# Two sequences' y turned to tokens by VectorE and through DRAM instead of by TensorE

## The chip, the cores and the metric

One core of one Trainium2 chip. The metric is the time of one execution on the device in microseconds (us); less is better. The core's engines work side by side, each through its own list of instructions in order, and meet only at semaphores: TensorE (PE: matmuls and transposes into PSUM; its weight loads are PEld), VectorE (DVE), ScalarE (ACT), GpSimd (POOL), and SyncE (SP), which here issues every DMA.

## The reference

Windowed attention, a gated layer that mixes tokens, and a mixer with a token layer and a channel layer. All float32, 4 sequences (b) of 576 tokens (s), 512 channels.

```python
# attention: 8 heads of 64, each token sees itself and the 63 before it
attn = softmax(where(mask, q @ k.T / 8, -1e9)) ; x = attn @ v          # (4, 576, 512)
# gated layer
h = relu(x @ w_in); u, v = h[..., :512], h[..., 512:]
v_n = (v - mean(v)) / sqrt(var(v) + 1e-6)
v_s = einsum('ts,bsd->btd', w_spatial, v_n) + b_spatial[None, :, None]
y = (u * v_s) @ w_out                                                   # (4, 576, 512)
# mixer
h = relu(y.transpose(0, 2, 1) @ w_tok1) @ w_tok2                        # over tokens
u2 = y + h.transpose(0, 2, 1)
out = u2 + relu(u2 @ w_ch1) @ w_ch2
```

The step that matters here: y comes out of `w_out` with its channels on the 128 partitions (4 tiles m of 128 channels, 576 tokens along the row), and the first token layer wants tokens on the partitions (5 tiles t, the last of 64 tokens, 512 channels along the row).

## The kernel before

**Arithmetic.** Nearly every product is made of three float32r matmuls on a high and a low part (high x high, high x low, low x high). ScalarE writes the high part of a value, VectorE (or GpSimd) the low part as value minus high part.

**Orders written out.** The work of each engine is a list of names, made of segments: a prologue (attention of sequence 0), a first turn (attention of sequence 1, everything behind it of sequence 0), `LOOP_...` twice (attention of sequence 2 with the rest of sequence 1, then attention of sequence 3 with the rest of sequence 2), and an epilogue. `order_of` turns names into entries; the kinds in `BACK` belong to the sequence before. A digit is a block, a tile, or a tile and a half of the tokens. SP has one list for all, `ALL_SP`, with the sequence as the first digit. In TensorE's list `+` is the second part of the unit before it, so that small pieces can stand between its parts.

**Names, in the order in which the work of a turn depends.** Attention, 9 blocks of 64 queries per sequence: `qt` (DVE turns q by 32x32 blocks; `kt` turns k), `S` (PE, scores), `m` (DVE, mask and maximum), `e` (ACT, exponent), `r` (DVE, inverse of the sum), `n` (POOL, normalise), `pt` (DVE, turn probabilities by 32x32 blocks), `pw` and `pr` (SP, store them to DRAM and load them back with the blocks rearranged: one store, four loads), `V` (PE, values), `o` (ACT, eviction to xT). `V` of a block waits for its `pr`; `pt` of a block waits for the `V` two before it. `lv`, `lk`, `lq` load v, k, q (16 DMAs each for k and q of a later sequence). `vo` copies a window of v. Then `xh`, `xl` (POOL, high and low part of x), `v` and `u` (PE, the two halves of `w_in`), `vr`, `vs`, `rs`, `vn`, `vh`, `vl` (normalising v), `uu` (ACT, u into the tile uy).
Behind it: `g` (PE, mixing over tokens), `sa`, `sm`, `gh`, `gl` (add bias, times u, high, low), `y` (PE, `w_out`), `yy` (ACT, y into uy), `t` (PE, y transposed: four 128x128 transposes of a tile into one PSUM bank), `th`, `tl` (ACT and DVE, high and low part of y by tokens), `a` (PE, first token layer, all tiles into two banks), `ah`, `al`, `b` (PE, second token layer), `te` (DVE, u2 = y + b in uy), `ut` (DVE, u2 turned by 32x32 blocks into `turn_at[m]`), `st` and `sr` (SP, u2 stored as it is, and as rows: the latter with four DMAs for each m that put the blocks in their places). `turn_at[3]` is the tile gate, so the first `sa` of the next turn waits for the last of the row stores.

**PSUM.** Four banks are handed round among the units `v`, `u`, `g`, `y`, `t`, `a`, `b`: a unit takes the bank used longest ago and waits until the unit before it there has been evicted (`take_acc`, `unit_free`).

**Lines.** L1291 is the product of three matmuls, L1392 the same for products over tokens (`over_tokens`: `g` and `a`), L1331 scores, L1361 values, L1310 and L1341 the prologue's transposes, L1380 those of the spatial weights, L1455 the transposes of y. L849 is `th`, L844 `yy`, L1118 `tl`, L1099 `sa`, L1024 `pt`, L1137 `ut`. SP's: L572 `pw`, L578 `pr`, L583 `sr`, L568 `st`, L502 the k and q loads of later sequences, L632 loads of u2 rows in the last stage (channel layer).

Of the kernel before, what the change touches and what calls it, by code (L numbers as in the profile page):

```python
# [25 lines left out]
def bass_attention_gmlp_mixer_kernel(nc, q, k, v, w_in, w_spatial, b_spatial, w_out, w_tok1, w_tok2, w_ch1, w_ch2, out):  # L26
# [21 lines left out]
    def tile_of(blk):  # L48
# [50 lines left out]
        "te30 te01 vn0 vs1 te11 vl0 te21 te31 vn1 ut0 vs2 ut1 vl1 vn2 vs3 vl2 vn3 ut2 ut3 vs4 kt0 vl3 vn4 kt1 vl4").split()  # L99
# [10 lines left out]
        "n0 n1 n2 n3 n4 xh0 n5 n6 xh1 xl0 n7 xl1 n8 xh2 xl2 rs0 rs1 xh3 xl3 xh4 xl4 rs2 rs3 rs4").split()  # L110
# [9 lines left out]
        "cw40 cw41 st30 st31 st32 st33 ca42 sr30 sr31 sr32 sr33").split()  # L120
# [23 lines left out]
    BACK = ("g", "y", "t", "a", "b", "sa", "sm", "gh", "gl", "yy", "th", "tl", "ah", "al", "te", "ut")  # L144
# [40 lines left out]
    with ctx:  # L185
# [144 lines left out]

        prob_dram = nc.dram_tensor("prob_blocks", (2, 4, P, P), F32, kind="Internal").ap()
# [19 lines left out]
        a_low = sem("a_low")  # L351
        w2_low = sem("w2_low")
# [77 lines left out]
        ODD = counts(DVE_ORDER, ("vo",))  # L430

# [321 lines left out]
        def _(act):  # L753
# [196 lines left out]
        def _(dve):  # L950
# [654 lines left out]
```

## Time and profile before

| | |
|---|---|
| time, median of 3 runs | 655.45 us (653.43 to 655.53) |
| the profiled execution | 653.59 us, of which the span of its instructions 651.0 us |
| granted clock of TensorE | 1.00 in the whole span |
| PE busy | 638.4 us, 98% of the span |
| DVE, ACT, POOL busy | 433.1, 297.8, 138.4 us |
| DMA | 76.76 MB over the one queue that SP fills, 45.2% of 16 engines' time |

The span runs from the first to the last instruction. Busy time leaves out waits and the issuing of DMAs. A chain that ended last is followed back from the last instruction, at each step to what released it. Rows of a timeline begin with the start and the length in us; `x4` is a count of instructions, and what stands in square brackets is idle time of the engine just before the row and what ended it.

### The profile page before, as it was taken

The page shows a single profiled execution, that of the slowest core. Times are in us where ns is not written, and L with a number is a line of the kernel's source. Part 1 is how long each engine was busy: PE and PEld are TensorE (multiplying, and loading weights), DVE is VectorE, ACT ScalarE, POOL GpSimd, SP SyncE. Part 2 cuts the span into 40 slices and gives each one's busy share as a digit, 9 for nine tenths or more (in the row PEclk, how much of TensorE's full clock was granted, in tenths as well). Part 3 has the DMA queues.
Part 4 walks back from the last instruction along what each step waited for, and adds up shares of the span by engine and source line. Part 5 has one row for each costly group of instructions (what it writes and reads, how often), then busy time and mean ns, then how long its engine had stood idle before and what let it go on. Part 6 is the DMA issues. An engine that isn't in the chain of part 4 may idle for free.

```text
span 651.0 us, 11538 instructions
## 1 busy us (share of the span) xinstructions
PE 638.4 (98%) x3917; PEld 589.1 (90%) x3917; DVE 433.1 (67%) x1073; ACT 297.8 (46%) x733; POOL 138.4 (21%) x232
## 2 busy tenths in 40 slices
PE   5899999999999999999999999999999999999997
PEld 5798999989998899988999989988898889889886
DVE  4988887666865778766473666776756775755534
ACT  4865447334464344652347334453334454243331
POOL 3561426531234304252107700000000000000000
PEclk9999999999999999999999999999999999999999
DMA  9858135586444883344730174252632332422412
GB/s 209 212 92 197 35 86 158 129 169 107 128 117 116 178 139 87 107 121 113 165 128 2 61 177 134 73 173 83 213 108 65 121 107 64 163 64 66 162 33 97
DMA packets 190872, 77.48 MB, mean 119 GB/s; under 512 B 127328, under 2 KB 177056, under 8 KB 190816
## 3 DMA queue, kind: packets, MB, share of 16 engines
q1 hardware_dynamic: 190816, 76.76, 45.2%
q8 instruction: 32, 0.52, 0.3%
q14 instruction: 24, 0.20, 0.1%
HBM read 55.49 MB, written 21.23 MB: 118 GB/s over the span
## 4 chain that ended last, share of the span: by engine, by line
PE 95%; DMA 2%; DVE 1%; POOL 1%; SPq 0%; issue 0%; ACT 0%; POOLq 0%; DVEq 0%
PE ps L1291 71%; PE ps L1392 13%; PE ps L1361 4%; PE ps L1331 4%; DMA early<-in_moe_w_spatial_dram 2%; PE ps L1455 1%; PE ps L1310 0%; PE ps L1380 0%; DMA out_dram<-front 0%; DVE front L1195 0%; PE ps L1341 0%; DVE att L995 0%; ACT att L763 0%; POOL att L675 0%; SPq L544 0%
## 5 line engine op out<-in xcount | busy, mean ns | idle before, releaser
L1291 PE MATMUL ps<-arena 128*128 128x288 f32 (+3 forms) x2100 | 396.3, 342 | 0.0
L1291 PEld LDWEIGHTS ps<-arena 128*128 128x128 f32 (+1 forms) x2100 | 335.2, 186 | 33.7
L1291 PE MATMUL ps<-att_r,arena 128*128 128x384 f32 x504 | 101.5, 336 | 0.0
L1291 PEld LDWEIGHTS ps<-att_r,arena 128*128 128x128 f32 x504 | 90.0, 188 | 7.1
L1392 PE MATMUL ps<-arena 128*128 128x288 f32 (+1 forms) x560 | 89.6, 316 | 0.0
L1392 PEld LDWEIGHTS ps<-arena 128*128 128x128 f32 x560 | 80.5, 188 | 4.1
L690 POOL TENSOR_SCALAR att<-att,rinv 128x128 f32<-128x128 f32 x144 | 53.8, 393 | 98.1 <-DVE rinv L1006 97.9
L783 ACT ACTIVATE att<-att,nmax 128x128 f32<-128x128 f32 x144 | 56.0, 392 | 25.8 <-DVE nmax L995 25.3
L881 ACT ACTIVATE xT<-ps 128x384 f32<-128x384 f32 x54 | 26.5, 491 | 52.1 <-PE ps L1291 52.1
L1171 DVE TENSOR_TENSOR arena<-front,arena 128x1792 fp32r<-128x1792 f32 x16 | 32.4, 2025 | 16.1 <-ACT arena L873 16.0
L1181 DVE TENSOR_TENSOR vr<-ps,xT 128x384 f32<-128x384 f32 x36 | 20.0, 556 | 31.7 <-PE ps L1291 25.0
L995 DVE CUSTOM_DVE_ANT_0 att<-ps,mask 128x128 f32<-128x128 f32 x144 | 33.1, 285 | 11.5 <-PE ps L1331 11.0
L893 ACT ACTIVATE arena<-vr 128x384 fp32r<-128x384 f32 x36 | 18.7, 520 | 43.8 <-PE ps L1291 35.7
L1331 PE MATMUL ps<-att 128*128 128x128 f32 x288 | 37.4, 280 | 0.9 <-DVE att L969 0.9
L1361 PE MATMUL ps<-att 128*128 128x128 f32 x288 | 37.1, 276 | 0.7 <-DVE att L969 0.4
L873 ACT ACTIVATE arena<-front 128x1792 fp32r<-128x1792 f32 x18 | 30.7, 1704 | 13.4 <-DVE front L1161 13.4
L1186 DVE SCALAR_TENSOR_TENSOR arena<-vr,arena 128x384 fp32r<-128x384 f32 x36 | 21.2, 589 | 23.3 <-ACT arena L893 23.3
L1331 PEld LDWEIGHTS ps<-att 128*128 128x128 f32 x288 | 35.4, 196 | 1.3 <-DVE att L969 1.2
L1361 PEld LDWEIGHTS ps<-att 128*128 128x128 f32 x288 | 34.7, 192 | 1.7 <-DVE att L969 0.6
L793 ACT ACTIVATE xT<-ps 64x256 f32<-64x256 f32 x72 | 27.1, 377 | 14.6 <-PE ps L1361 13.6
L893 ACT ACTIVATE arena<-xT 128x384 fp32r<-128x384 f32 x18 | 9.5, 525 | 48.4 <-PE ps L1291 32.7
L1129 DVE TENSOR_TENSOR uy<-ps,uy 128x288 f32<-128x288 f32 x32 | 14.2, 454 | 20.4 <-PE ps L1291 20.3
(101 smaller groups left out, 651.8 us busy)
## 6 DMA issues: line engine op xcount, KB each, us to landing
front<-in_moe_w_ch_dram SPq DMA_DIRECT2D x18, 512.0 KB, 4.7
prob_blocks<-att SPq DMA_DIRECT2D x27, 256.0 KB, 2.5
att<-prob_blocks SPq DMA_DIRECT2D x108, 64.0 KB, 2.0
u_scratch<-uy SPq DMA_DIRECT2D x16, 288.0 KB, 2.9
front<-in_moe_w_ch_dram SPq DMA_DIRECT2D x18, 256.0 KB, 2.9
front<-in_moe_w_ch_dram SPq DMA_DIRECT2D x36, 128.0 KB, 3.5
early<-u_rows SPq DMA_DIRECT2D x18, 256.0 KB, 5.6
att<-in_v_dram SPq DMA_DIRECT2D x16, 256.0 KB, 3.8
```

Source lines behind the costliest of these rows:

```text
L690: ins = pool.tensor_scalar(x, x, rinv[:, g % 3, p:p + 1], 1.0, ALU.mult, ALU.mult)
L783: ins = act.activation(x, x, ACT.Exp, bias=nmax[:, g % 3, p:p + 1], scale=-1.0, accum_out=psums[:, g % 3, p:p + 1])
L793: ins = act.activation(xT3[c, :, blk * WINDOW:(blk + 1) * WINDOW], tp[c, bank, :].rearrange("p (w h n) -> p w h n", w=PAIRS, h=2)[:, :, h, ...
L873: act.activation(a_hi_at[n % 2], a_raw[n % 2], ACT.Copy).then_inc(a_hi, 1)
L881: act.activation(part[x], ps[:, 6, 0:CK], ACT.Copy).then_inc(part_copied, 1)
L893: act.activation(h_at[:, j, 0], total[i], ACT.Relu).then_inc(h_hi, 1)
L995: ins = dve.tensor_tensor_reduce(out=prob[:, g % 3, P * p:P * (p + 1)], in0=ps[:, 4 + g % 2, P * p:P * (p + 1)], in1=mask[:, 0:P] if blk e ...
L1171: dve.tensor_tensor(a_lo_at[n % 2], a_raw[n % 2], a_hi_at[n % 2].bitcast(F32), ALU.subtract).then_inc(a_low, 1)
L1291: ins = pe.matmul(dst, w[a], x[c], start=first and n == 0, stop=last and n == 2, skip_group_check=True)
L1331: ins = pe.matmul(ps[:, 4 + g % 2, P * p:P * (p + 1)], qd[:, g // 2 % 2, g % 2, p].rearrange("p h n -> p (h n)"), kT[:, p, at:at + P], sta ...
L1361: ins = pe.matmul(tp[:, bank, P * p:P * (p + 1)], window[:, P * p:P * (p + 1)], keys[:, p], start=True, stop=True)
L1392: ins = pe.matmul(dst, d, w, start=t == 0 and n == 0, stop=t == NT - 1 and n == len(pairs) - 1, skip_group_check=True)
```

## The change

Sequences 1 and 2 (second and third, `TURNED`) no longer have `t` in TensorE's list. In its place: `ty` (DVE turns the 576 columns of uy's tile m by 32x32 blocks into `turn_at[m]`), `yw` (SP, four DMAs for each m that store the blocks to rows of `y_dram`, 72 KB each in pieces of 128 B), `yr` (SP, one DMA for each tile t that loads rows of 2 KB into `raw_y`, once all of y is stored and the last `g` is done). `raw_y` lies where the low part of vn lies, so `tl` works in place. `th` and `tl` read it instead of PSUM. The first sequence and the fourth keep TensorE's transposes. The orders of both loop turns are written anew for all engines, and `ALL_SP` from its start. The prologue, first turn and epilogue of the other engines are unchanged.

```diff
     LOOP_PE = (
-        "g00 S0 S1 + g10 S2 S3 + g20 + g30 + g01 + g11 + g21 + g31 S4 S5 V0 V1 + y00 + y10 + y20 + y30 + y01 S6 "
-        "V2 t0 + y11 + y21 + y31 + t1 S7 V3 t2 S8 V4 t3 t4 a0 a1 a2 a3 v0 a4 V5 V6 + v1 + b00 b10 b20 b30 b01 b11 "
-        "V7 V8 b21 v2 + b31 v3 + v4 + u00 + u10 + u20 + u30 + u01 + u11 + u21 + u31 +").split()
+        "S0 S1 g00 + g10 S2 + g20 + g30 + g01 + g11 + S3 S4 V0 g21 + g31 + y00 + y10 + V1 S5 V2 y20 + y30 + y01 + "
+        "y11 + S6 V3 y21 + y31 + V4 S7 v0 + S8 v1 V5 + a0 a1 a2 a3 a4 V6 v2 + b00 b10 b20 b30 b01 V7 b11 b21 V8 "
+        "b31 v3 + v4 + u00 + u10 + u20 + u30 + u01 + u11 + u21 + u31 +").split()
...
     LOOP_ACT = (
...
+        "e0 e1 e2 gh00 gh10 gh20 gh30 e3 gh01 e4 o0 gh11 gh21 yy00 yy10 gh31 o1 yy20 yy30 yy01 e5 yy11 o2 yy21 o3 "
+        "yy31 e6 e7 vr0 o4 th0 th1 o5 th2 th3 th4 vr1 e8 ah0 ah1 vh0 o6 vr2 o7 o8 vh1 vh2 vr3 uu00 vr4 uu10 vh3 "
+        "uu20 uu30 uu01 vh4 uu11 uu21 uu31").split()
...
     LOOP_DVE = (
...
+        "qt0 qt1 qt2 m0 qt3 m1 qt4 r0 m2 sa00 r1 pt0 sa10 sm00 sm10 pt1 gl00 gl10 sa20 sa30 sm20 r2 qt5 m3 sm30 "
+        "gl20 pt2 sa01 gl30 sm01 r3 m4 sa11 vo1 gl01 r4 sa21 sm11 pt3 sm21 gl11 pt4 sa31 sm31 gl21 gl31 qt6 m5 "
+        "ty0 vo2 r5 ty1 m6 pt5 ty2 qt7 ty3 qt8 r6 m7 pt6 r7 m8 vs0 tl0 tl1 pt7 tl2 tl3 tl4 vo3 vn0 r8 al0 al1 pt8 "
+        "vl0 vs1 te00 vn1 te10 te20 te30 te01 vo4 te11 kt0 te21 te31 ut0 ut1 vs2 vn2 ut2 vl1 vl2 vs3 ut3 vs4 kt1 "
+        "vn3 vn4 vl3 vl4").split()
...
     LOOP_POOL = (
-        "n0 n1 n2 n3 n4 xh0 n5 n6 xh1 xl0 n7 xl1 n8 xh2 xl2 rs0 rs1 xh3 xl3 xh4 xl4 rs2 rs3 rs4").split()
+        "n0 n1 n2 n3 n4 n5 xh0 xl0 xh1 n6 xl1 n7 xh2 rs0 xl2 n8 rs1 xh3 xl3 xh4 xl4 rs2 rs3 rs4").split()
...
     ALL_SP = (
-        "lq00 lk00 lq01 lv00 lv01 lk01 lq02 lk02 lw01 lq03 lk03 lv02 lw00 lw02 lz04 lv03 lk10 lv04 lq10 lw06 lv10 "
...
+        "lq00 lk00 lq01 lv00 lk01 lv01 lq02 lk02 lw01 lq03 lv02 lk03 lw00 lw02 lv03 lz04 lv04 lk10 lq10 lw04 lw06 "
...
+        "pw17 pw18 pr17 pr18 lk20 st00 st01 st02 st03 lq20 sr00 sr01 sr02 sr03 pw20 lv20 pr20 pw21 lv21 pw22 pr21 "
+        "pr22 lv22 pw23 pw24 pr23 pr24 yw10 lv23 yw11 pw25 yw12 yw13 pr25 pw26 yr10 yr11 yr12 yr13 yr14 pr26 pw27 "
+        "lk30 pw28 pr27 lv24 pr28 st10 lq30 st11 sr10 st12 st13 sr11 sr12 lv30 sr13 pw30 pr30 pw31 lv31 pw32 pr31 "
+        "pr32 pw33 pw34 lv32 pr33 pr34 yw20 yw21 pw35 yw22 yw23 pr35 yr20 yr21 yr22 yr23 yr24 pw36 lv33 pr36 pw37 "
+        "lv34 pr37 pw38 pr38 st20 st21 st22 cx40 cx41 cx42 sr20 st23 cx43 sr21 sr22 sr23 ca40 ca41 cw40 st30 st31 "
+        "sr30 sr31 sr32 sr33 ca42 st32 st33 cw41").split()
...
+                if kind == "yw":
+                    sp.wait_ge(y_turned, Y_TURNED["ty", b, x])
+                    for i in range(4):
+                        sp.dma_start(y_dram[b % 2, :, x * P + 32 * i:x * P + 32 * i + 32].rearrange("(j p) n -> p j n", p=32),
+                                     turn_at[x][32 * i:32 * i + 32, :].rearrange("p (j n) -> p j n", n=32)).then_inc(y_stored[x], 16)
+                if kind == "yr":
+                    if x == 0:
+                        for m in range(KD):
+                            sp.wait_ge(y_stored[m], 64 * b)
+                        sp.wait_ge(*unit_full(("g", b, 31)))
+                    sp.dma_start(raw_y[0:rows(x), 1, x], y_dram[b % 2, toks(x), :]).then_inc(y_in[x], 16)
...
             def yt_high(b, t):
                 r = rows(t)
-                act.wait_ge(*unit_full(("t", b, t)))
-                act.activation(vn[0:r, 0, t, :], ps[0:r, BANK_OF["t", b, t], :], ACT.Copy).then_inc(yt_hi, 1)
+                if b in TURNED:
+                    act.wait_ge(y_in[t], 16 * b)
+                    src = raw_y[0:r, 1, t]
+                else:
+                    act.wait_ge(*unit_full(("t", b, t)))
+                    src = ps[0:r, BANK_OF["t", b, t], :]
+                act.activation(vn[0:r, 0, t, :], src, ACT.Copy).then_inc(yt_hi, 1)
...
+            def turn_y(b, m):
+                dve.wait_ge(rows_stored[m], 64 * b)
+                apart(dve)
+                dve.wait_ge(*unit_free(("y", b, 10 * m + 1)))
+                dve.transpose(turn_at[m], uy3[:, m, :]).then_inc(y_turned, 1)
```

## Rows read from the trace of the kernel before

**Rows 1.** The page: busy times, GB/s of 40 slices, chain by engine

```profile
PE 638.4 (98%) x3917; PEld 589.1 (90%) x3917; DVE 433.1 (67%) x1073; ACT 297.8 (46%) x733; POOL 138.4 (21%) x232
...
GB/s 209 212 92 197 35 86 158 129 169 107 128 117 116 178 139 87 107 121 113 165 128 2 61 177 134 73 173 83 213 108 65 121 107 64 163 64 66 162 33 97
...
PE 95%; DMA 2%; DVE 1%; POOL 1%; SPq 0%; issue 0%; ACT 0%; POOLq 0%; DVEq 0%
```

**Rows 2.** The chain in order of time, third sequence's turn (start, length)

```profile
152.61 1.18 PE ps L1392 x9
...
159.21 11.15 PE ps L1392 x84
...
172.14 1.79 PE ps L1361 x16
...
183.50 0.44 PE ps L1455 x4
183.94 5.60 PE ps L1291 x42
...
194.86 5.49 PE ps L1392 x24
...
204.41 8.88 PE ps L1291 x54
...
237.66 1.18 PE ps L1392 x9
```

**Rows 3.** TensorE's timeline of the start

```profile
12.45 0.66 PE L1310 MATMUL ps<-ident,att 128*128 128x128 f32 x4 [0.99 <-DMA att<-in_k_dram]
...
30.05 1.09 PE L1380 MATMUL ps<-ident,early 128*128 128x128 f32 x8 [0.33 <-DMA early<-in_moe_w_spatial_dram]
```

**Rows 4.** VectorE's groups by form, 150 to 240 us (busy us, mean ns)

```profile
L1118 DVE TENSOR_TENSOR arena<-ps,arena 128x512 fp32r<-128x512 f32 x4 | 2.7, 684 | 2.0 <-ACT arena L849 2.0
...
L1137 DVE STREAM_TRANSPOSE early<-uy 128x576 f32<-128x576 f32 x3 | 2.3, 775 | 0.0
```

**Rows 5.** VectorE's timeline, start of the same turn

```profile
161.98 0.46 DVE L1099 TENSOR_TENSOR gate<-ps,bias 128x288 f32<-128x288 f32 x1 [0.99 <-DMA u_rows<-gate]
162.36 0.70 DVE L1024 STREAM_TRANSPOSE att<-att 128x512 f32<-128x512 f32 x1
```

**Rows 6.** SP's timeline, 125 to 182 us (length is that of the issues)

```profile
126.99 9.36 SPq L502 DMA_DIRECT2D att<-in_k_dram  x16
...
138.50 10.63 SPq L502 DMA_DIRECT2D att<-in_q_dram  x16
149.18 6.62 SPq L583 DMA_DIRECT2D u_rows<-early  x12
...
163.08 0.38 SPq L572 DMA_DIRECT2D prob_blocks<-att  x1
...
165.61 3.88 SPq L578 DMA_DIRECT2D att<-prob_blocks  x8
```

**Rows 7.** DMA issues, 150 to 240 us (KB each, median us to landing)

```profile
prob_blocks<-att SPq DMA_DIRECT2D x9, 256.0 KB, 2.5
att<-prob_blocks SPq DMA_DIRECT2D x36, 64.0 KB, 2.0
u_rows<-early SPq DMA_DIRECT2D x23, 72.0 KB, 2.1
att<-in_v_dram SPq DMA_DIRECT2D x5, 256.0 KB, 3.4
```

**Rows 8.** The page's DMA issues, of the last stage

```profile
front<-in_moe_w_ch_dram SPq DMA_DIRECT2D x18, 256.0 KB, 2.9
...
early<-u_rows SPq DMA_DIRECT2D x18, 256.0 KB, 5.6
```

**Rows 9.** ScalarE's groups by form, 150 to 240 us

```profile
L844 ACT ACTIVATE uy<-ps 128x288 f32<-128x288 f32 x8 | 3.3, 408 | 3.4 <-PE ps L1291 3.4
...
L849 ACT ACTIVATE arena<-ps 128x512 fp32r<-128x512 f32 x4 | 2.4, 597 | 2.6 <-PE ps L1455 2.6
```

More of the change, by code:

```diff
@@ L78, in bass_attention_gmlp_mixer_kernel @@
     LOOP_ACT = (
-        "e0 e1 e2 gh00 gh10 gh20 e3 gh30 gh01 e4 gh11 yy00 o0 o1 yy10 yy20 gh21 gh31 yy30 o2 yy01 th0 e5 yy11 e6 "
-        "yy21 yy31 th1 th2 o3 th3 e7 o4 e8 th4 ah0 o5 ah1 vr0 o6 vr1 vh0 o7 o8 vr2 vh1 vr3 vh2 uu00 vr4 vh3 uu10 "
-        "uu20 uu30 uu01 uu11 vh4 uu21 uu31").split()
+        "e0 e1 e2 gh00 gh10 gh20 gh30 e3 gh01 e4 o0 gh11 gh21 yy00 yy10 gh31 o1 yy20 yy30 yy01 e5 yy11 o2 yy21 o3 "
+        "yy31 e6 e7 vr0 o4 th0 th1 o5 th2 th3 th4 vr1 e8 ah0 ah1 vh0 o6 vr2 o7 o8 vh1 vh2 vr3 uu00 vr4 uu10 vh3 "
+        "uu20 uu30 uu01 vh4 uu11 uu21 uu31").split()
     EPILOGUE_ACT = (
@@ L95, in bass_attention_gmlp_mixer_kernel @@
     LOOP_DVE = (
[3 rows of a table removed]
-        "te30 te01 vn0 vs1 te11 vl0 te21 te31 vn1 ut0 vs2 ut1 vl1 vn2 vs3 vl2 vn3 ut2 ut3 vs4 kt0 vl3 vn4 kt1 vl4").split()
[4 rows of a table added]
+        "vn3 vn4 vl3 vl4").split()
     EPILOGUE_DVE = (
@@ L113, in bass_attention_gmlp_mixer_kernel @@
     ALL_SP = (
[6 rows of a table removed]
-        "cw40 cw41 st30 st31 st32 st33 ca42 sr30 sr31 sr32 sr33").split()
[7 rows of a table added]
+        "sr30 sr31 sr32 sr33 ca42 st32 st33 cw41").split()
     SEGMENTS = {"PE": [PROLOGUE_PE, FIRST_PE, LOOP_PE, LOOP_PE, EPILOGUE_PE], "ACT": [PROLOGUE_ACT, FIRST_ACT, LOOP_ACT, LOOP_ACT, EPILOGUE_ACT],
@@ L143, in bass_attention_gmlp_mixer_kernel @@
     AHEAD = ("kt",)
-    BACK = ("g", "y", "t", "a", "b", "sa", "sm", "gh", "gl", "yy", "th", "tl", "ah", "al", "te", "ut")
+    BACK = ("g", "y", "t", "a", "b", "sa", "sm", "gh", "gl", "yy", "th", "tl", "ah", "al", "te", "ut", "ty")
     PE_ORDER, ACT_ORDER, DVE_ORDER, POOL_ORDER = (order_of(e) for e in ("PE", "ACT", "DVE", "POOL"))
@@ L329, in bass_attention_gmlp_mixer_kernel @@
         rows_dram = nc.dram_tensor("u2_rows", (B * S, DM), F32, kind="Internal").ap()
+        y_dram = nc.dram_tensor("y_rows", (2, S, DM), F32, kind="Internal").ap()
         prob_dram = nc.dram_tensor("prob_blocks", (2, 4, P, P), F32, kind="Internal").ap()
@@ L351, in bass_attention_gmlp_mixer_kernel @@
         a_low = sem("a_low")
+        y_turned = sem("y_turned")
+        y_stored = [sem(f"y_stored{i}") for i in range(KD)]
+        y_in = [sem(f"y_in{i}") for i in range(NT)]
         w2_low = sem("w2_low")
@@ L430, in bass_attention_gmlp_mixer_kernel @@
         ODD = counts(DVE_ORDER, ("vo",))
+        Y_TURNED = counts(DVE_ORDER, ("ty",))
+        TURNED = (1, 2)
+        raw_y = early[:, START["vn"] - START["w_out"]:START["tok2"] - START["w_out"]].rearrange("p (s t n) -> p s t n", s=2, t=NT)
         def unit_full(u):
@@ L856, in token_high @@
                     for m in range(3):
-                        act.wait_ge(rows_stored[m], 64 * b)
+                        if b in TURNED:
+                            act.wait_ge(y_stored[m], 64 * b)
+                        else:
+                            act.wait_ge(rows_stored[m], 64 * b)
                 act.wait_ge(*unit_full(("acc_a", b, c)))
@@ L1117, in yt_low @@
                 dve.wait_ge(yt_hi, YT_HI["th", b, t])
-                dve.tensor_tensor(vn_low(t), ps[0:r, BANK_OF["t", b, t], :], vn[0:r, 0, t, :].bitcast(F32), ALU.subtract) \
+                src = raw_y[0:r, 1, t] if b in TURNED else ps[0:r, BANK_OF["t", b, t], :]
+                dve.tensor_tensor(vn_low(t), src, vn[0:r, 0, t, :].bitcast(F32), ALU.subtract) \
                     .then_inc(acc_dve, 1)
@@ L1135, in turn_residual @@
                     dve.wait_ge(rows_stored[m], 64 * b)
+                if b in TURNED:
+                    dve.wait_ge(y_stored[m], 64 * b)
                 dve.wait_ge(acc_dve, ACC_DVE["te", b, 10 * m + 1])
@@ L1217, in _ @@
                     spatial_lo(x)
+                elif kind == "ty":
+                    turn_y(b, x)
                 elif kind == "vs":
```

9 rows, old and new, of tables (ALL_SP, LOOP_DVE) are left out of this document.

## The prediction, made before the change was run

> **What bounds the kernel now.** I read the page first, for the busy shares and the chain that ended last. TensorE is busy 638.4 of 651.0 us and the chain is 95% its own work [rows 1]: any instruction taken off TensorE is worth its full time, and any wait put before it costs its full time, unless something else is already late. Second, the chain of waits in order of time, over the turn of the loop in which attention of the third sequence is woven with the gated and token layers of the second [rows 2]: from 152.61 to 237.66 us there is no piece that isn't TensorE's. I count times in a turn from its start (+0 is 152.61). The same rows price TensorE's pieces: a tile's four y transposes 0.44, one block of scores or values 0.89 (x16 is two blocks), a `g` unit of 14 matmuls 1.86 (11.15 x 14 / 84), a `y` or `u` unit of 12 matmuls 1.60, less in longer rows (I take 1.58), a `b` unit half of that, a `v` unit 2.73 and a step of `a` 1.37, its last somewhat less. Third, TensorE's timeline of the start, where its few waits are [rows 3]. Then I walk the other engines in their new written order, with the durations of the rows below.
>
> **What goes.** Ten tiles of y (five in each of two turns) lose their four transposes: 10 x 0.44 = 4.4 us less on TensorE [rows 2]. ScalarE's and VectorE's evictions stay in number, with another source. By itself this is -4.4 us.
>
> **What comes, and where it lies.** For each of two sequences: 4 block transposes on VectorE of 0.78 us [rows 4] = 3.1 us; 16 stores of 72 KB and 5 loads of up to 256 KB on SP's queue. An issue of the same stores took 6.62 / 12 = 0.55 us [rows 6], of the loads about 0.44 (a 256 KB store's 0.38 and a 64 KB load's 0.485 are the nearest rows [rows 6]). That is 16 x 0.55 + 5 x 0.44 = 11 us more in SP's order per turn. VectorE has room in sum, SP too; what counts is each due time on TensorE.
>
> **Place 1: the first values block, turn one.** `V0` stood at +19.5 [rows 2]; in the new order it stands after 6 `g` units and 5 blocks of scores: 6 x 1.86 + 5 x 0.89 = +15.6. What feeds it doesn't move. `pt0` stands behind `sa00` on VectorE, and `sa00` is held by the previous sequence's last row store until 161.98 us (+9.4), by a wait of 0.99 us [rows 5]. The work before that point is untouched, so `pt0` again ends near +10.85 (now r1's two small instructions are ahead of it too); `pw20` is issued at +10.9; its read-back may go 2.53 us later (165.61 - 163.08 [rows 6]), at +13.4; the fourth of its loads is issued 3 x 0.485 later and lands 2.0 us after that [rows 6, 7]: +16.9. A wait of 1.3 us, where before 2.5 us were to spare. Bounds 1.0 (shortest landings) to 1.5. Queued behind `V0` is all of TensorE. `g01`, due at +10.1, needs `sa00`, done at +9.85: it just passes. In turn two the row stores were issued much earlier, so neither binds.
>
> **Place 2: y to tokens.** Between the end of `y31` and `a0` TensorE has `V4 S7 v0 S8 v1 V5`: 4 x 0.89 + 2 x 2.73 = 9.0 us. In turn one `y31` ends at +38.7 (with place 1's wait) and `a0` is due at +47.8. The chain: eviction by ScalarE 0.41 [rows 9], `ty3` 0.78 behind `qt7`, done at +40.05. SP is later than that: it waits for the third sequence's `ty1` and `ty2`, and `pw25` lies between, so `yw12` is issued from +38.5, `yw13` from +40.6 to +42.7. Then `pr25` (four issues, 1.75) and `pw26` (0.4) stand ahead of `yr10`: +44.85. The last store landed (2.1 after its issue [rows 7]) at +44.3, so the queue, not the landing, sets it. The load is 256 KB: the nearest rows are 2.9 us for a load of that size with long rows and 3.4 with short ones [rows 7, 8]; I take 2.9, then `th0` 0.60 [rows 9] and `tl0` 0.68 [rows 4]: `a0` can start at +49.2, a wait of **1.4 us**. `V5`, due 1.4 us before it, also waits for `pr25` about 0.6 us, which is inside the same 1.4. Later tiles come 0.44 to 0.7 us apart, `a` steps take 1.37, so no further wait. In turn two there is no `pw36` ahead of the loads: `yr20` goes at +43.05, `a0` could start at +47.35 against +46.35 due: **1.0 us**. Bounds for each: a landing of 2.0 (the shortest kind, 64 KB) takes 0.9 off; one of 5.6, as the same rows-to-tokens loads took in the last stage, where six queued behind each other and behind weights [rows 8], adds 2.7. I stand by 2.9 because here the queue is drained before them.
>
> [...]
>
> **Place 3: `V7` and `V8`, turn one.** The k load of the next sequence, 16 DMAs that took SP 9.36 us [rows 6], moves ahead of `pw28` and `pr27`. `pt7` waits for `tl1`, so `pw27` goes at +50.6 and the k load from +51.0 to about +60.2; `pw28` +60.6, `pr27` to +62.3, landed +63.9. `V7` is due at +63.3: 0.6. `pr28` follows by 2.5 and the `V` before it by one more wait of about 0.1. I take 0.7; bounds 0 and 1.8 (landings of 3 us behind that burst). In turn two the k load isn't there: 0.
>
> **Place 4: the start.** SP's first loads change order too. `lv01` now lies between the k and q tiles that TensorE waits for (0.99 us, for the third k tile), which may cost up to 1.2 (its 256 KB at the 212 GB/s of that slice [rows 1]); `lv02` moves ahead of `lk03`, so the spatial weights are asked for 0.6 us sooner, which can give back the 0.33 wait [rows 3]. Together 0, bounds -0.3 and +1.2.
>
> **Hidden.** The q load now lies ahead of the u2 stores `st11` to `st13` in turn one (16 issues, 10.6 us [rows 6]): `uu10` comes about 2 us late, but its bank is needed only 2.5 us after that; by my walk `u31` has 1.5 us to spare. `sa31`, due for the bank of `y30`, has 0.25 us. If that cover is gone, each costs what it is late. GpSimd's new order lets `xh0` wait for `y31` before `n6`; `n6` is still done before `pt6` is wanted. The order written for TensorE from 322.70 us on is the same.
>
> **The sum.** -4.4 + 1.3 + 1.4 + 1.0 + 0.7 + 0 = 0.0 us (with each wait at its least, 0.3 + 1.8 + 0.7 + 0.3 lower, -3.1; at its most, 0.2 + 5.4 + 1.1 + 1.2 higher, +7.9). Against the profiled execution's own 653.59 us (a span of 651.0 and 2.6 around it) that is 653.6. The median shown is 655.45, two runs near 655.5 and one at 653.43, so the profiled one was among the quick ones; I put the sum on the median: 655.4 us. 0.3%, or 2.0 us, is about what a measurement can tell from no change.
>
> **The rivals.**
> *A, the trip is hidden and the gain is kept (faster).* If the y stores go at 0.40 apiece (a single issue took 0.38 [rows 6]) instead of 0.55, the eight of `yw12` and `yw13` save 1.2 us and `yr10` goes at +43.6; with a landing of 2.5, as the 256 KB store's, `a0` is on time in both turns. If the row store behind `sa00` also lands 0.6 us sooner, place 1 is halved. -4.4 + 0.7 + 0 + 0 + 0.3 is -3.4: 652.0. For it: TensorE shows no wait in the old turns, so waits of this kind were avoided throughout. Against it: the +9.4 release and the 2.53 us between store and read-back are rows, not guesses. It decides from a sum of waits under 2.4 us.
> *B, the loads of y queue (slower).* All five loads are issued at once, 1.2 MB, and the first shares the engines with them, with `pr25` and with the last stores. If the first lands after 5.6 us as in [rows 8], each `a0` waits 2.7 us more: 0.0 + 5.4 = 660.8; with 4.2 us, 658.0. It decides from a landing of 3.9 us. For it: that very kind of load has no shorter row. Against it: those stood behind 1.5 MB of weights.
> The Trainium skill (VectorE: DVE Perf Modes, Rules for kernel authors) advises TensorE for a 128x128 transpose and VectorE only for 32x32 ones; it points to B's side, and no row here decides it.
> *C, nothing is taken off the path.* It would need TensorE to idle where the transposes stood; it doesn't [rows 1, 2], so only the waits above can eat the gain.
>
> **Chances.** No measurable change, the sum as it stands, 0.50. A, faster, 0.28. Slower 0.22: B with 0.15, late covers (`u31`, `y30`, place 3 at its bound) 0.07. The range takes in A whole and B up to a landing of about 4.4 us: 651.0 to 658.5, which leaves out less than 2 in 10. My own likeliest case spans 653.5 to 657.4.
>
> **What would show it.** Right: L1455 falls from 80 to 40 matmuls; VectorE has 8 more transposes of 128x576; in TensorE's waits, one of about 1.3 us on the att load before `V0` only in turn one, two of 1 to 1.5 us on VectorE's low part before `a0`, one under 1 us before `V7`; both turns of about equal length as before, the first some 1 us longer, the second 1 us shorter. Wrong: a y load that lands in over 4 us or under 2.5, no wait at `V0`, or a wait in the run of `u` units.

## The result: 2.4% slower

| | before | after |
|---|---|---|
| time, median of 6 runs each | 653.08 us (651.71 to 655.53) | 669.51 us (668.01 to 670.2) |
| ratio, 95% interval | | 1.0241 [1.0216, 1.0266] |
| the profiled execution | 653.59 us, span 651.0 | 669.25 us, span 667.4 |
| TensorE busy | 638.4 us | 639.2 us |
| mean granted clock | 1.00 | 0.994 |

The change costs 16.4 us; the forecast was 655.4 us with a range to 658.5. The page of the changed kernel answers to [rows 1]: busy times of the engines, GB/s of 40 slices, the chain by engine.

```profile
PE 639.2 (96%) x3877; PEld 586.3 (88%) x3877; DVE 444.0 (67%) x1081; ACT 298.7 (45%) x733; POOL 138.4 (21%) x232
...
GB/s 212 208 106 170 32 100 166 114 180 115 147 143 195 156 117 111 149 183 199 139 35 1 59 222 84 63 159 73 211 126 88 85 143 64 156 66 64 157 32 95
...
PE 78%; SPq 9%; DMA 7%; DVE 2%; issue 2%; ACT 2%; POOL 1%; DVEq 0%; POOLq 0%; ACTq 0%
```

Forty matmuls are gone and eight block transposes are there, as the change says, yet TensorE is busy for no less time: a part ran at half clock (below), and a piece right behind a wait counts longer (1.16 for 1.05). The chain was 95% TensorE's and is now 78%; SP's issuing (SPq), which had 0%, has 9%. So the place to look is SP's queue. TensorE's timeline says where the time went. I cut it at TensorE's first unit of each turn (the first `g` in the old order, the first scores in the new one) and at the start of the epilogue.

| stretch | before | after | difference | predicted |
|---|---|---|---|---|
| start to turn one | 152.45 | 152.47 | 0.0 | 0 |
| turn one | 85.05 | 90.04 | +5.0 | +1.2 |
| turn two | 85.05 | 85.59 | +0.5 | -1.2 |
| epilogue to the end of the span | 328.5 | 339.3 | +10.8 | 0 |

**Turn one.** TensorE's timeline of the changed kernel, the middle of the turn (L1402 values, L1372 scores, L1332 three-part products, L1433 products over tokens, here `a`; a wait of the row stands in square brackets):

```profile
190.75 1.06 PE L1372 MATMUL ps<-att 128*128 128x128 f32 x8
192.26 3.02 PE L1332 MATMUL ps<-arena 128*128 128x512 f32 x12 [0.45 <-POOL arena L730]
...
200.31 1.16 PE L1402 MATMUL ps<-att 128*128 128x128 f32 x8 [2.76 <-DMA att<-prob_blocks]
...
203.70 4.66 PE L1433 MATMUL ps<-arena 128*128 128x512 f32 x18 [0.84 <-DVE arena L1149]
208.90 2.58 PE L1433 MATMUL ps<-arena 128*128 128x512 f32 x10 [0.54 <-DVE arena L1149]
...
222.49 1.16 PE L1402 MATMUL ps<-att 128*128 128x128 f32 x8 [0.71 <-DMA att<-prob_blocks]
```

The largest wait is not `a0`'s for y (0.84) but that of `V5` for its probabilities, 2.76 us, shortly before it. SP's timeline of the same kernel shows why (start and length of the issues; L594 is `yw`, the y stores, L589 `pr`, L583 `pw`, L601 `yr`, L550 `lv`):

```profile
184.73 3.38 SPq L594 DMA_DIRECT2D y_rows<-early  x4
188.21 0.46 SPq L550 DMA_DIRECT2D att<-in_v_dram  x1
188.71 2.47 SPq L594 DMA_DIRECT2D y_rows<-early  x4
191.22 0.51 SPq L583 DMA_DIRECT2D prob_blocks<-att  x1
191.78 2.65 SPq L594 DMA_DIRECT2D y_rows<-early  x4
194.47 2.21 SPq L594 DMA_DIRECT2D y_rows<-gate  x4
196.73 1.96 SPq L589 DMA_DIRECT2D att<-prob_blocks  x4
198.73 0.43 SPq L583 DMA_DIRECT2D prob_blocks<-att  x1
199.34 2.36 SPq L601 DMA_DIRECT2D early<-y_rows  x5
```

From 184.7 us on SP does nothing but issue. `pw25` went at 191.22, and its read-back could have gone some 2.5 us later (as `pr20` did behind `pw20`), but the eight stores `yw12` and `yw13` stand between them and hold it until 196.73. The sixteen stores took 10.7 us, not 8.8: 0.84 each for the first four as a mean, then 0.62, 0.66, 0.55. Then the loads of y: ScalarE's timeline (L876, `th`), with what it waited for.

```profile
202.29 0.63 ACT L876 ACTIVATE arena<-early 128x512 fp32r<-128x512 f32 x1 [5.66 <-DMA early<-y_rows]
203.75 0.63 ACT L876 ACTIVATE arena<-early 128x512 fp32r<-128x512 f32 x1 [0.83 <-DMA early<-y_rows]
```

The first load landed 2.9 us after its issue, as I took it; the other four, all five issued within 2.36 us, landed 4.0, 4.6, 5.7 and 5.6 us after their issues, so up to 1.6 us apart, and that is the 0.54 before a later step of `a`.

**Turn two** has only 0.45 at `v0` and 1.15 at `V5`; no `pw36` lies ahead of its y loads.

**Last stage.** The chain of waits in order of time, start and length, where the last stage (L1332 again) stops:

```profile
371.92 6.29 PE ps L1332 x43
...
379.08 0.78 DVE early L1176
...
379.88 0.32 SPq L605
...
388.32 0.53 SPq L605
...
388.95 0.48 SPq L617
...
390.03 3.43 DMA front<-in_moe_w_ch_dram
...
395.07 1.70 ACT arena L903
396.77 0.39 ACT xT L911
...
397.30 6.78 PE ps L1332 x26
```

Read from its end: TensorE waits 7.58 us (390 to 397) for ScalarE (L911), which stands behind the high part of channel weights (L903), which waits for VectorE's sums of them, and these for three loads, issued from 388.95 on (the last at 390.03) behind sixteen row stores `sr30` to `sr33` (L605), the first of which waited for u2 of the last sequence turned by VectorE, done at 379.86. Before, the same weights (`ca42`, L595 to L597) had gone ahead of the row stores. SP's timeline of the kernel before:

```profile
373.64 0.41 SPq L595 DMA_DIRECT2D front<-in_moe_w_ch_dram  x1
374.10 0.57 SPq L596 DMA_DIRECT2D front<-in_moe_w_ch_dram  x1
374.72 0.46 SPq L597 DMA_DIRECT2D front<-in_moe_w_ch_dram  x1
375.22 7.29 SPq L583 DMA_DIRECT2D u_rows<-early  x12
```

That is one edit at the very end of `ALL_SP`: its first row store stands 88 us behind the last `a0` that reads a y from DRAM (291.37). The windows of the changed kernel there (busy us and instructions of PE, PEld, DVE, ACT, POOL; then clock, DMA share, GB/s):

```profile
388.00:392.00 4.00, 1.72 (x8) 1.10 (x7) 0.00 (x0) 0.00 (x0) 0.00 (x0) 1.00 0.72 166
392.00:396.00 4.00, 0.00 (x0) 0.00 (x0) 1.52 (x4) 0.93 (x1) 0.00 (x0) 0.70 0.91 295
396.00:400.00 4.00, 2.71 (x8) 2.64 (x9) 2.60 (x3) 2.77 (x5) 0.00 (x0) 0.50 0.89 281
400.00:404.00 4.00, 4.00 (x20) 3.59 (x20) 2.74 (x5) 0.76 (x2) 0.00 (x0) 0.94 0.37 131
```

After 7.6 us of idleness TensorE resumes at a granted clock of 0.50, 1.2 GHz, and is back near full speed in the next window. From the start of the epilogue to the end of TensorE's last matmul lie 335.8 us against 325.0: 10.8, of which 7.58 is this wait, 1.26 another at 588.56 (below), and most of the rest, 2.0, the slow clock: the first two groups behind the wait (397.30 to 401.25) took 3.95 us in place of 2.43.

### The profile page after: what moved, and what is told of

It reads as the page before. It is cut to its first block, busy times and chain, and to the rows that moved or that the text cites. A ratio compares the mean times of both kernels' runs of the same rounds, so it can differ in the third digit from the quotient of the medians.

```text
span 667.4 us, 11510 instructions
## 1 busy us (share of the span) xinstructions
PE 639.2 (96%) x3877; PEld 586.3 (88%) x3877; DVE 444.0 (67%) x1081; ACT 298.7 (45%) x733; POOL 138.4 (21%) x232
## 4 chain that ended last, share of the span: by engine, by line
PE 78%; SPq 9%; DMA 7%; DVE 2%; issue 2%; ACT 2%; POOL 1%; DVEq 0%; POOLq 0%; ACTq 0%
PE ps L1332 59%; PE ps L1433 11%; PE ps L1402 3%; SPq L594 3%; PE ps L1372 3%; SPq L589 2%; DMA prob_blocks<-att 2%; DMA front<-in_moe_w_ch_dram 1%; DMA early<-in_moe_w_in_dram 1%; SPq L605 1%; SPq L513 1%; DMA early<-y_rows 1%; DMA att<-prob_blocks 1%; DVE front L1234 1%; PE ps L1382 1%
## 5 line engine op out<-in xcount | busy, mean ns | idle before, releaser
L1332 PE MATMUL ps<-arena 128*128 128x288 f32 (+3 forms) x2100 | 399.3, 343 | 0.9 <-POOL arena L730 0.9
L1332 PEld LDWEIGHTS ps<-arena 128*128 128x128 f32 (+1 forms) x2100 | 335.5, 187 | 34.9 <-POOL arena L730 1.3
L1332 PE MATMUL ps<-att_r,arena 128*128 128x384 f32 x504 | 102.7, 339 | 8.8 <-ACT xT L911 8.8
L1332 PEld LDWEIGHTS ps<-att_r,arena 128*128 128x128 f32 x504 | 90.7, 189 | 16.5 <-issue 9.7
L1433 PE MATMUL ps<-arena 128*128 128x288 f32 (+1 forms) x560 | 89.6, 316 | 1.5 <-DVE arena L1149 1.4
L1433 PEld LDWEIGHTS ps<-arena 128*128 128x128 f32 x560 | 80.2, 188 | 7.2 <-DVE arena L1149 3.3
L805 ACT ACTIVATE att<-att,nmax 128x128 f32<-128x128 f32 x144 | 56.2, 392 | 23.5 <-DVE nmax L1025 23.1
L911 ACT ACTIVATE xT<-ps 128x384 f32<-128x384 f32 x54 | 26.6, 492 | 52.6 <-PE ps L1332 52.6
L1402 PE MATMUL ps<-att 128*128 128x128 f32 x288 | 38.4, 277 | 5.4 <-DMA att<-prob_blocks 5.1
L1402 PEld LDWEIGHTS ps<-att 128*128 128x128 f32 x288 | 35.3, 191 | 7.7 <-DMA att<-prob_blocks 6.6
L903 ACT ACTIVATE arena<-front 128x1792 fp32r<-128x1792 f32 x18 | 30.7, 1704 | 22.8 <-DVE front L1200 22.8
L1372 PE MATMUL ps<-att 128*128 128x128 f32 x288 | 38.4, 283 | 0.6 <-DVE att L999 0.6
L1372 PEld LDWEIGHTS ps<-att 128*128 128x128 f32 x288 | 36.4, 199 | 1.1 <-DVE att L999 0.8
L861 ACT ACTIVATE arena<-gate 128x288 fp32r<-128x288 f32 x32 | 13.8, 445 | 31.7 <-DVE gate L1136 31.6
```

Source lines behind the costliest of these rows:

```text
L805: ins = act.activation(x, x, ACT.Exp, bias=nmax[:, g % 3, p:p + 1], scale=-1.0, accum_out=psums[:, g % 3, p:p + 1])
L903: act.activation(a_hi_at[n % 2], a_raw[n % 2], ACT.Copy).then_inc(a_hi, 1)
L911: act.activation(part[x], ps[:, 6, 0:CK], ACT.Copy).then_inc(part_copied, 1)
L1332: ins = pe.matmul(dst, w[a], x[c], start=first and n == 0, stop=last and n == 2, skip_group_check=True)
L1372: ins = pe.matmul(ps[:, 4 + g % 2, P * p:P * (p + 1)], qd[:, g // 2 % 2, g % 2, p].rearrange("p h n -> p (h n)"), kT[:, p, at:at + P], sta ...
L1402: ins = pe.matmul(tp[:, bank, P * p:P * (p + 1)], window[:, P * p:P * (p + 1)], keys[:, p], start=True, stop=True)
```

## The experiments

Theories at the start. T1: SP's order is the cause, in two places: its end (the 9 to 10 us of the last stage) and the y stores ahead of `pr25` and the y loads (turns one and two). T2, the rival: the cost lies in the trip itself, its landings and the memory traffic, and in the turns' other new orders, so restoring one piece of SP's list gives little. All times are medians; ratios are to the kernel before on the same chip, with a 95% interval.

**1. The changed kernel with the old end of SP's list.**

```diff
-... ca40 ca41 cw40 st30 st31 sr30 sr31 sr32 sr33 ca42 st32 st33 cw41
+... ca40 ca41 cw40 cw41 st30 st31 st32 st33 ca42 sr30 sr31 sr32 sr33
```

> The changed kernel with only the end of SP's list put back: st30 to st33 and then ca42 (the third set of channel weights) ahead of the sixteen row stores sr30 to sr33. Theory (late weights): the last stage lost 10.9 us because ca42 stood behind the row stores; of it 7.6 us are the wait at 389.7 us, about 2 the half clock after it, 1.3 a second weight load at 587 us. Expected 658.6 to 660 us, 9.6 to 10.9 less than the changed kernel, about 1.008 to 1.010 of the kernel before. Rival (the trip through DRAM itself delays the last stage, by DMA traffic or by the last turn): no more than 3 us come back, 666 to 670.

Measured: 659.69 us (657.62 to 660.66), 1.0096 [1.0065, 1.0127]. Epilogue and last stage take 325.0 us again, the clock is 0.999. So the end of the list was 9.8 of the 16.4 us, as expected, and 6.4 are left: turn one 89.4 us, turn two 86.9. (Turn two had 85.6 in the changed kernel's profile, with the same orders: a turn moves by over 1 us from one profile to the next.) The edit also moves `cw41`, `st32` and `st33`; it is `ca42` that the chain above names.

**2. The kernel before with only the new end of SP's list** (the same words the other way round, y still transposed by TensorE).

> The kernel before with only the end of SP's list as in the changed kernel: ca42 behind sr33, st32 st33 cw41 last; nothing of y is changed. Theory (late weights): it alone costs 9.6 to 10.9 us, 663 to 664.5, with one wait of 7 to 8 us before the second group of hidden units and a half clock of TensorE after it. Rival (it needs the new turns): no change, 653.

Measured: 662.19 us (661.86 to 662.58), 1.0136 [1.0118, 1.0153]: +8.9, somewhat less than expected. TensorE's timeline of this kernel:

```profile
381.19 1.22 PE L1291 MATMUL ps<-att_r,arena 128*128 128x384 f32 x6
382.25 1.55 PE L1291 MATMUL ps<-arena 128*128 128x512 f32 x6
391.22 2.26 PE L1291 MATMUL ps<-att_r,arena 128*128 128x384 f32 x6 [7.42 <-ACT xT L881]
393.28 2.03 PE L1291 MATMUL ps<-arena 128*128 128x512 f32 x6
395.15 1.22 PE L1291 MATMUL ps<-att_r,arena 128*128 128x384 f32 x6
```

The same wait without anything of y's trip, and the price of the clock in plain sight: six matmuls that took 1.22 us take 2.26 right after the wait, and the next six 2.03 instead of 1.55; the rows after are normal. Its epilogue and last stage are 9.2 us longer: 7.42 and 1.7 more, 1.5 of it in the two groups right behind the wait. T1 holds for this place, from both sides.

**3 and 4. One turn of each kind** (both with the old end): the y trip and the new orders in one turn, the kernel before's orders and TensorE's transposes in the other.

```diff
-        TURNED = (1, 2)
+        TURNED = (2,)         # run 3: only turn two is new
...
+        TURNED = (1,)         # run 4: only turn one is new
```

> End of SP's list as before; the first of the two loop turns with the old orders and TensorE's transposes, the second with the new orders and the trip through DRAM (third sequence only). Theory (two costs, one for each turn, that don't depend on each other): +0.5 us against before, as the trace of the changed kernel has 85.6 us for that turn against 85.05, so 653.5 to 654. Rival (a turn in the new order pays for what the first new turn left late): the second turn alone would gain up to 2.2, 651.

> The mirror of e3: only the first loop turn new (second sequence's y through DRAM), the second turn and the end of SP's list old. Theory: +5.0 us against before (90.04 against 85.05 us for that turn), 658 to 658.5. Rival (the wait before a0 is a chance of the profiled run): between 0 and +2.5.

Measured: turn two alone 656.16 us (655.61 to 658.32), 1.005 [1.0031, 1.007]; turn one alone 659.31 us (657.7 to 662.28), 1.0097 [1.0063, 1.013]. In the profiles turn one is 4.5 us longer where it alone is new (89.5), turn two 1.15 longer where it alone is (86.2), and the old turn beside it keeps its 85.0. Both came out above what I expected, and turn two's trip isn't free. The profile of run 3 has a wait of 2.24 us at 402.46 in the last stage as well, on weights that landed late (8.5 us for 128 KB), and epilogue and last stage are 4.0 us longer there; that of run 4 has one of 0.98 at 404.46.

Run 4's TensorE timeline shows a second price of a wait in the turn:

```profile
199.16 2.08 PE L1418 MATMUL ps<-att 128*128 128x128 f32 x8 [2.25 <-DMA att<-prob_blocks]
200.88 2.33 PE L1348 MATMUL ps<-arena 128*128 128x512 f32 x6
```

The same two pieces took 1.16 and 1.64 behind `V5`'s wait in the changed kernel. The granted clock of this stretch is 0.70 (200 to 204 us), against 1.00 there, though the changed kernel waited longer, 2.76. So waits of this size sometimes bring the half level and sometimes don't: in run 4 three of four executions had a mean clock of 0.995 to 0.997, in run 3 one of five, in run 1 two of four; before is at 0.999 to 1.00 throughout. The losses of the halves sum to 8.8 us in place of 6.4. Such episodes can't explain all of it: in run 3 four of five executions, the median among them, had a clock of 1.00. The intervals of the three runs, about 1.3, 2.2 and 2.0 us to either side, barely leave room for no difference; the rest stays open.

**5. The orders alone.** Everything of run 1, but no `ty`, `yw`, `yr`; TensorE's transposes are put into its new list.

```diff
-y11 + S6 V3 y21 + y31 + V4 S7 v0 + S8 v1 V5 + a0 a1 a2 a3 a4 V6 ...
+y11 + S6 V3 y21 + y31 + V4 t0 S7 t1 v0 t2 + S8 v1 V5 + t3 t4 a0 a1 a2 a3 a4 V6 ...
```

> The new orders of both turns, end of SP's list as before, but y of the second and third sequence transposed by TensorE as before (t0, t1, t2 among V4, S7, v0; t3, t4 ahead of a0), with no trip through DRAM. Theory (the new orders by themselves cost next to nothing, the trip costs it): 653.5 to 655, with v0 and V7, V8 waiting 0.5 to 1.5 us in all. Rival (the new orders are worse whatever carries y): 657 or more.

Measured: 654.25 us (653.58 to 657.3), 1.0014 [1.0003, 1.0025]. Both turns take 85.66 us with no wait that the timeline names; 0.6 more than the old ones. (The profile is that of the slowest execution, 657.3 us; its epilogue and last stage are 3.0 us longer than before's.) By the interval the new orders cost 0.2 to 1.6 us.

**6. The orders, the block transposes and the stores of y, read by nobody.** Run 5 and `ty` and `yw`; `yr` is left out, and `th` and `tl` read TensorE's transposes. It prices VectorE's and SP's load without the dependence of `a` on it (`ah0` and `ut` still wait until the stores have landed, as in the changed kernel).

```diff
+ty0 vo2 r5 ty1 m6 pt5 ty2 qt7 ty3 tl0 ...             # VectorE
+... yw10 lv23 yw11 pw25 yw12 yw13 pr25 pw26 pr26 ...  # SP
```

> As e6, and VectorE also turns y by blocks and SP also stores it to DRAM (16 stores for each of the two sequences), which nothing reads; the tokens come from TensorE's transposes. It separates the load on SP's queue from the wait for the trip. Theory (SP's queue holds up the probabilities' loads behind the stores): a wait before V5 of 1 to 1.5 us in the first turn and up to 0.5 in the second, 1 to 2 us over e6. Rival (only the dependence of a0 on the trip costs): the same as e6.

Measured: 656.98 us (656.16 to 659.25), 1.0055 [1.0038, 1.0073]: 2.7 us above run 5, more than either side expected. In its profile (again the slowest execution) turn one takes 88.2 us and turn two 86.1. TensorE's timeline of it, where the large wait was:

```profile
199.16 1.16 PE L1402 MATMUL ps<-att 128*128 128x128 f32 x8 [1.03 <-DMA att<-prob_blocks]
...
219.79 1.16 PE L1402 MATMUL ps<-att 128*128 128x128 f32 x8 [0.69 <-DMA att<-prob_blocks]
```

and `V5` in TensorE's timeline of run 5:

```profile
197.99 1.05 PE L1401 MATMUL ps<-att 128*128 128x128 f32 x8
```

`V5` waits for `pr25` although nothing of the attention depends on y: the stores delay it by sitting ahead of it in SP's queue. `pr25` was issued at 195.57 us, in run 5 at 190.27, and landed 1.9 to 2.2 us after its issues, no later than elsewhere. The stores also load the DMA engines, which are 82% busy from 184 to 196 us for 150 GB/s; without the stores (run 5) 29% for 79 GB/s.

**7. A second queue for the last y stores.** Half of `yw2` and `yw3` issued by ScalarE, and the y loads ahead of `pw26`.

```diff
-for i in range(4):                     # SP
+for i in range(4 if x < 2 else 2):
...
+yy31 yw2 yw3 e6 e7 vr0 ...             # ScalarE issues i = 2, 3
...
-yw12 yw13 pr25 pw26 yr10 yr11 yr12 yr13 yr14 pr26
+yw12 yw13 pr25 yr10 yr11 yr12 yr13 yr14 pw26 pr26
```

> As e1 (end of SP's list restored), and of the stores of y those of the last two channel tiles shared out: two of four on SP's queue, two on ScalarE's, with the y loads now ahead of pw26. Theory (the trip is late because SP issues sixteen stores one after another at about 0.6 us): the y loads go 3 us sooner in the first turn, the values block V5 no longer waits (2.5 us in e1), a0 waits about 1 us; turns of 86.2 and 84.1 us, 653.5 in all. Rival (the landing of the five loads behind each other sets a0 and a3, whenever they are issued): V5's wait goes, but as much comes back at a0 and a3, 656 to 657.

Measured: 664.38 us (661.84 to 666.05), 1.0164 [1.0143, 1.0186]: 4.7 us worse than run 1 where a gain was expected. `V5` and `a0` no longer wait, as I wanted. But two other waits of turn one, 2.21 us at `v1` (for `xl1`) and 2.98 at `V7`, were each followed by a stretch at half clock, here the second one in TensorE's timeline:

```profile
220.18 2.08 PE L1410 MATMUL ps<-att 128*128 128x128 f32 x8 [2.98 <-DMA att<-prob_blocks]
221.91 3.23 PE L1340 MATMUL ps<-arena 128*128 128x288 f32 x12
```

The twelve matmuls took 1.84 us at full clock in the changed kernel. The mean clock was 0.991 to 0.995 in all five executions. Both waits are explained with the next run, which has them too.

**8. Every y store split between both queues.** As run 7, with half of each `yw`, and ScalarE's earlier in its order.

> As e5 with all four tiles' stores shared between SP's and ScalarE's queue, eight issues each. Theory: y loads go near 195 us in the first turn, a0 is on time; what is left of waits are v0 on GpSimd's low part (0.45 in each turn) and V7, V8 (0.85 in the first). 650.5 to 651.5, 0.996 to 0.997 of the kernel before: this is the version that could beat it. Rival (the trip's landings): 654 or more. A second rival: ScalarE is held by the issues, yy and e6 come late, and a wait of 1 us or more shows before V6 or S8.

Measured: 660.3 us (659.34 to 662.26), 1.011 [1.0092, 1.0128]. What I wanted happened: SP issues the y loads at 196.42, 2.9 us sooner than in the changed kernel, and neither `a0` nor `V5` waits in turn one. ScalarE's timeline tells what it cost (ACTq is ScalarE's DMA issues; L805 is `e`):

```profile
189.94 1.21 ACTq L871 DMA_DIRECT2D y_rows<-early  x2
191.19 2.08 ACTq L871 DMA_DIRECT2D y_rows<-gate  x2
193.32 0.40 ACT L805 ACTIVATE att<-att,nmax 128x128 f32<-128x128 f32 x1 [2.97 <-issue]
```

and TensorE's where it arrives:

```profile
192.13 3.06 PE L1340 MATMUL ps<-arena 128*128 128x512 f32 x12 [0.45 <-POOL arena L730]
...
198.30 1.65 PE L1340 MATMUL ps<-arena 128*128 128x512 f32 x6 [2.22 <-POOL arena L730]
...
220.75 1.16 PE L1410 MATMUL ps<-att 128*128 128x128 f32 x8 [4.20 <-DMA att<-prob_blocks]
```

`e6` stands 2.97 us behind ScalarE's issues; `n6` is late by it, and behind `n6` in GpSimd's order stands `xl1`, for which `v1` waits 2.22 us. The wait of `V7` comes from `pw26`, which now stands behind the y loads: issued at 198.76, it landed 5.3 us later (in run 7 5.2; ahead of the loads 2.7 in the changed kernel and 2.8 in run 1). SP waited for it until 204.13 before it could issue `pr26`, so `pw27` and the sixteen k loads (206.39 to 215.06) went no sooner than in the changed kernel, though TensorE was 2.5 us ahead; `pr27` was issued at 216.76 in place of 215.44, and `V7` waits 4.20 us, with a granted clock of 0.50 from 222 to 224. The second rival's mechanism, ScalarE held by its issues, came true, with the wait at `v1`; the late `pw26` was in no expectation.

**9. The k and q loads moved out of the way.** The k load of the next sequence behind `pr28`, the q load issued by ScalarE late in the turn.

```diff
-pw27 lk30 pw28 pr27 lv24 pr28 st10 lq30 st11 ...
+pw27 pr27 pw28 lv24 pr28 lk30 st10 st11 ...           # the q load by ScalarE
```

> As e1 with only the k and q loads of the next sequence changed as in e9; y stores all on SP. Theory (the k load ahead of pw28 costs what e1's profile shows at V7 and V8): 0.85 us less than e1, 658.5 to 659, all in the first turn. Rival: q on ScalarE's queue delays uu and costs 1 us or more.

Measured: 660.23 us (658.13 to 661.79), 1.0104 [1.0084, 1.0125]: no gain over run 1 where 0.85 us was expected. `V7` no longer waits, but `V0` waits 0.48, `V8` 0.87 and a `u` unit 0.60.

**10. Run 9, and some of the y stores to ScalarE (`yw0` whole, `yw1` half), `xl1` ahead of `n6`.**

> A version made from what e1, e5 and e7 showed: end of SP's list as before; of the y stores, tile 0 and half of tile 1 on ScalarE's queue while it is idle, the rest on SP; GpSimd's xl1 ahead of n6; the next sequence's k load behind pr28, its q load (16 DMAs) on ScalarE's queue in pairs among its later work. Theory (each wait was SP's queue, or an engine held by issues): v1 no longer waits on GpSimd (2.2 us in e7), V7 no longer behind the k load (4.2 in e7), a0 waits under 1 us, v0 0.45 in each turn. 650 to 651.5, 0.995 to 0.997. Rival (the trip's own latency, two landings in a row and the loads that share the engines, leaves 1.5 to 2 us at a0 and a3 in each turn): 653 to 655, no gain over the kernel before.

Measured: 662.99 us (660.15 to 664.65), 1.0141 [1.0113, 1.017]. It was to be the version that beats both kernels, and even its rival (653 to 655) was too low. In turn one most of the waits that I went for became smaller (`V5` 1.55 against 2.51 in run 1; none at `v0`, `v1` or `V7`), `a0`'s did not (1.02 against 0.80), and others came. TensorE's timeline:

```profile
191.12 1.16 PE L1391 MATMUL ps<-att 128*128 128x128 f32 x8 [0.74 <-DVE att L1027]
...
202.42 6.64 PE L1452 MATMUL ps<-arena 128*128 128x512 f32 x28 [1.02 <-DVE arena L1168]
...
233.61 9.76 PE L1351 MATMUL ps<-arena 128*128 128x288 f32 x60 [2.18 <-ACT vr L843]
```

The granted clock is 0.62 from 234 to 238 us, behind the last. The 2.18 us comes from the moved k load: sixteen issues from 215.66 on now last 11.67 us, the stores of u2 stand behind them, and ScalarE waits 4.52 us for one of those before it may overwrite uy. No version that I ran beats the kernel before.

Of the two theories, T1 holds at the end of SP's list (runs 1 and 2) and for `pr25` behind the y stores (run 6). T2 has a part as well: run 5 prices the new orders at 0.7 us, and runs 7 and 8 show a landing that the trip's own loads delay.

## Why the prediction was wrong

**The step that failed: "Hidden", its last sentence.** It says that the order written for TensorE from 322.70 us on is the same, and the sum takes that as a last stage of the same length. TensorE's order is the same; SP's isn't, and the diff shows it: `ca42` behind `sr30` to `sr33`. Most of it could have been read from before's trace: those row stores took 7.3 and 2.2 us of issues from 375.22 on, so a load behind them goes 9.5 us later; the high part of these weights was done at 381.30 and the group of matmuls that needs it began at 384.01, so 2.7 us were to spare, and a wait of 6.8 us is an estimate from these rows (7.58 measured). I walked SP's list in turn one and not its end. This was 9.8 us of 16.4 (run 1 against the changed kernel), 8.9 by itself (run 2). It was none of the rivals; "an edit far from the place that the change is about" was in no chance.

**"What goes", 4.4 us:** right in number (L1455, now L1496, from 80 matmuls to 40). The bill of the rest, without the end, follows from runs 5, 6 and 1, each against the kernel before on its chip (+0.7, +3.4, +6.4): orders 0.7, VectorE's and SP's load 2.7, then the dependence on the trip in place of the transposes 3.0. The last holds the 4.4 us that the transposes give back, so depending on the trip costs about 7.4 by itself, and the trip with its load 10.1 for 4.4 gained. The turns in the profiles of these runs give 1.2, 3.0 and 2.0 for the three; the step from run 6 to run 1 is the least sure, as their intervals (1.0038 to 1.0073 and 1.0065 to 1.0127) touch.

**Place 1:** predicted 1.3, measured 0. The mechanism is there, but with no room to spare: `sa00` could begin at 160.49 instead of 161.98 [rows 5] (the last row store was issued at 158.4 and landed some 2 us later), so `pw20` went at 161.92, at +9.45 in place of +10.9, its read-back 2.55 us later (2.53 predicted), and `V0` at 168.04 found its data. Rival A's remark, that this landing could come sooner, was right. In run 9 `V0` waited 0.48.

**Place 2:** predicted 1.4 and 1.0 in all; measured 2.76 + 0.84 + 0.54 and 1.15. The duration of the y load was right (2.9), the queue in front of it wasn't: 10.7 us for the sixteen stores in place of 8.8, and the y loads at 199.34 in place of 197.3. The wait appears mostly at `V5`, which I had put at 0.6 inside `a0`'s: `pr25` is behind the same stores. The spacing of the later tiles, up to 1.6 us in place of 0.44 to 0.7, added 0.54.

The Trainium skill (DMA: Bandwidth & Descriptors, Issuing engines are not separate DMA queues) says that DMAs of all issuers run on the same 16 engines, so a second issuer saves only issue time, which it calls usually small. The first half fits what run 8 shows: with two queues issuing y stores these landed 3.8 us after their issues as a median, with one queue (the changed kernel) 2.6. The second is no guide here: one issue took 0.55 to 0.84 us beside that landing of 2.6, and sixteen in a row held a queue on which the attention depends for 10.7 us.

**Place 3:** predicted 0.7, measured 0.71, though at `V8` and not at `V7`. **Place 4:** 0 predicted, 0.0 measured (152.47 against 152.45). The wait of 0.33 [rows 3] is gone, and one of 0.45 at 107.83 came.

**Not foreseen:** `v0` waits 0.45 us in both turns for GpSimd's low part of x (L730), which ends at 192.21. I had followed `n6` in GpSimd's new order and not `xl0`.

**The rivals.** B (the y loads queue) had the right sign and the wrong place: the first load didn't land late, the later ones did (4.0 to 5.7), worth 0.54 us. Where `pw26` stood behind them (runs 7 and 8) they cost more. A asked for waits under 2.4 us; those named in the two turns alone sum to 6.9. C's condition, that nothing leaves the path, did not arise.

## What to carry to other kernels

When a diff rewrites the order of a shared DMA queue, compare old and new lists word by word to their end, and ask of each load that moved what it now stands behind and until when that waits: one group of loads moved behind stores that wait for the last result cost more than all of the rest. Price a detour through memory by the issues it puts ahead of others' short loads, and by what its own loads do to the landings behind them, not by its own landing alone. And where several engines work close to their due times, moving a piece out of one queue mostly moves the wait: of four attempts here to improve the trip, none gained.

## What the runs showed of the hardware

- The same kind of store (72 KB in pieces of 128 B) took SP 0.54 to 0.66 us to issue, as means of four, and once 0.84; in runs 7 and 8, where ScalarE issued such stores beside SP, means of two were up to 1.04 us on ScalarE's queue (2.08 for two) and up to 1.14 on SP's.
- Four issues on ScalarE's queue (3.3 us) held up its compute behind them: 2.97 us before `e6` in run 8, 2.96 in run 7.
- Five loads issued back to back landed 2.9, 4.0, 4.6, 5.7 and 5.6 us after their issues (256 KB each, the last 128), and a store of 256 KB issued right behind five such loads after 5.2 and 5.3 us (runs 7 and 8), in place of 2.7 and 2.8 ahead of them.
- After an idle stretch of 7.4 to 7.6 us the granted clock was at 0.50, the level of 1.2 GHz, for some 4 us after the work resumed; six matmuls took 2.26 in place of 1.22 us. Waits of 2.2 to 4.2 us were followed by the same level in the profiles of runs 3, 4, 7, 8 and 10, and waits of 2.51 us in run 1, 2.76 in the changed kernel's turn one and 2.22 in run 8 were not. In run 3 the two groups behind the wait of 2.24 us took 4.07 in place of 2.43 us: 1.6 us on top of the wait.
- Open: loads of channel weights of 128 KB landed after 3.4 us as a median and after 5.5 to 8.5 us at times (8.5 in run 3, where it was issued right behind loads of u2), with waits of 0.2 to 2.2 us on TensorE in the last stage that differ from kernel to kernel (2.24 in run 3; 1.26 at 588.56 in the changed kernel, behind a load of 5.46). What sets them, and what decides whether the clock falls after a wait of 2 to 3 us, I did not test; differences below 2 us between these runs aren't put down to one cause. Open too: the changed kernel's turn one is 5.0 us longer where its waits named by the timeline, less the 2.2 us of transposes, give 3.1, and the orders alone 0.6; 1.3 are in pieces too short to show.
